# Seven half-size products in place of eight in one block of a split-precision MLP layer

## The chip, the cores and the metric

One NeuronCore of one Trainium2 chip runs the whole program in one launch. The metric is the device time of that launch in microseconds. All arrays come in and go out as fp32.

## What is computed

The reference has three stages. The change lies in the MLP of the second one:

```python
    X = np.fft.fft(x, axis=1)
    X = np.fft.fft(X, axis=2)
    mixed = np.real(X).astype(np.float32)
    u = x + mixed
    mu = np.mean(u, axis=-1, keepdims=True)
    var = np.mean((u - mu) ** 2, axis=-1, keepdims=True)
    un = (u - mu) / np.sqrt(var + 1e-06)
    ch = np.maximum(un @ w_ch1, 0.0) @ w_ch2
    return (u + ch).astype(np.float32)
```

Here x is 2 x 768 x 512 and comes from a block-wise linear attention of 8 heads. w_ch1 is 512 x 2048 and w_ch2 is 2048 x 512. The third stage is a causal convolution gate of 5 taps and two 512 x 512 products.

## The kernel before

Everything is kept transposed: features on the 128 partitions, tokens along the free dimension. The program writes the instruction list of each engine by hand and orders the engines by semaphores.

**Precision.** Each fp32 operand of a large product is split into a rounded high part (an fp32r copy by ScalarE) and a low part (the difference). A product is three matmuls: high x high, low x high, high x low.

**Tiles.** The 1536 tokens form three blocks (`tb`) of 512. The 2048 hidden features form 8 groups (`g`) of 256. A step `m` is one group of one block, so there are 24 steps: 0 to 7 for block 0, 8 to 15 for the middle block, 16 to 23 for block 2.

**TensorE.** `mlp_hidden` (L558) of step m makes 256 hidden features x 512 tokens in banks ps0 and ps1: 2 halves of 12 matmuls with 512 columns. `mlp_out` (L583) of step m makes 4 x 6 matmuls with 512 columns that accumulate in ps4 to ps7 over the 8 groups of a block. In `mlp_step` (L637) the layer 1 of step m+1 is issued ahead of the layer 2 of step m. Banks ps2 and ps3 are free in the MLP but for the Fourier transforms of batch 1 (steps 0 to 3), `mean` and `variance` (L545). The variances of pieces 2 and 3 stand in step 9.

**ScalarE** (`mlp_step`, L858). `hidden_hi` (L799) writes relu(hidden) as fp32r to `hh`. `second_hi` (L767) and `first_hi` (L757) make the high parts of the weights, two and three steps ahead. `cen_hi` (L791) does so for the centred tokens. `squares` (L774), `squares_hi` and `inverse_root` (L784: Ln and Exp, each behind a load of its table) serve the variances.

**VectorE** (`mlp_step`, L1203). `hidden_lo` (L1093) writes the low part of relu(hidden) to `hl`. `centre` (L1060) subtracts the mean. `add_eps` (L1069) reads a variance out of ps2 or ps3, and its semaphore `s_ve` says that the bank is free. `newton` (L1073) refines the inverse root by three instructions on 768 columns. `finish` (L1101) scales the block's result and adds it to `u`.

**GpSimd** makes the low parts of the weights (`first_lo` L1296, `second_lo` L1301), half of those of the centred tokens (`cen_lo` L1306), and `square_sum` and `squares_lo`.

**SyncE** issues the weight loads, each into one of two raw buffers once the splits of that buffer are through.

The lines of layer 1 for one half, with its waits:

```python
                        mm(bank[:, :], w1h[st.slot][:, r, cols], xh, start=r == 0, stop=False)
                        mm(bank[:, :], w1l[st.slot][:, r, cols], xh, start=False, stop=False)
...
                        m = mm(bank[:, :], w1h[st.slot][:, r, cols], cen_l[st.tb][:, r], start=False, stop=r == R - 1)
```

## Time and profile before

| | us |
|---|---|
| median of 3 runs | 429.46 (429.06 to 429.52) |
| the profiled execution, its own time | 428.87 |
| its span, first to last instruction | 426.8 |
| TensorE matmul busy | 421.7 (99% of the span) |
| TensorE weight loads busy | 349.5 (82%) |
| VectorE / ScalarE / GpSimd busy | 244.2 / 173.3 / 189.7 |

An instruction's row in the timeline has its start, its duration, engine, line, operation, operands and count. An ended idle time and its releaser stand in brackets. Matmuls overlap: the distance from one start to the next is what a matmul costs, and its duration is longer. A wait on a semaphore that is already satisfied does not show.

### The profile page before, as it was taken

The page shows a single profiled execution, that of the slowest core. Times are in us where ns is not written, and L with a number is a line of the kernel's source. Part 1 is how long each engine was busy: PE and PEld are TensorE (multiplying, and loading weights), DVE is VectorE, ACT ScalarE, POOL GpSimd, SP SyncE. Part 2 cuts the span into 40 slices and gives each one's busy share as a digit, 9 for nine tenths or more (in the row PEclk, how much of TensorE's full clock was granted, in tenths as well). Part 3 has the DMA queues.
Part 4 walks back from the last instruction along what each step waited for, and adds up shares of the span by engine and source line. Part 5 has one row for each costly group of instructions (what it writes and reads, how often), then busy time and mean ns, then how long its engine had stood idle before and what let it go on. Part 6 is the DMA issues. An engine that isn't in the chain of part 4 may idle for free.

```text
span 426.8 us, 6315 instructions
## 1 busy us (share of the span) xinstructions
PE 421.7 (99%) x2482; PEld 349.5 (82%) x2482; DVE 244.2 (57%) x371; ACT 173.3 (41%) x318; POOL 189.7 (44%) x115
## 2 busy tenths in 40 slices
PE   8999999999999999999999999999999999999997
PEld 7888888788888788888888888888888888888886
DVE  5659999758446341971417101516988859669400
ACT  2355842675203327524262222264254342624212
POOL 3553322344886346986645444445545338300000
PEclk9999999999999999999999999999999999999999
DMA  7987701420331132223232322222321221002022
GB/s 251 356 330 237 224 2 56 141 102 20 129 98 50 51 100 98 98 72 126 93 104 75 117 91 89 89 88 84 105 75 38 99 91 49 0 0 100 0 100 98
DMA packets 14860, 44.06 MB, mean 103 GB/s; under 512 B 1904, under 2 KB 2160, under 8 KB 14832
## 3 DMA queue, kind: packets, MB, share of 16 engines
q1 hardware_dynamic: 14832, 43.67, 30.1%
q8 instruction: 20, 0.33, 0.3%
q14 instruction: 8, 0.07, 0.0%
HBM read 40.52 MB, written 3.15 MB: 102 GB/s over the span
## 4 chain that ended last, share of the span: by engine, by line
PE 96%; DMA 2%; SPq 1%; DVE 1%; ACT 0%; issue 0%
PE ps L572 10%; PE ps L598 10%; PE ps L600 10%; PE ps L599 10%; PE ps L580 10%; PE ps L573 10%; PE ps L487 3%; PE ps L700 3%; PE ps L699 3%; PE ps L698 3%; PE ps L676 3%; PE ps L449 3%; PE ps L677 3%; PE ps L678 3%; PE ps L476 2%; PE ps L531 2%
## 5 line engine op out<-in xcount | busy, mean ns | idle before, releaser
L1097 DVE SCALAR_TENSOR_TENSOR hl<-ps,hh 128x512 fp32r<-128x512 f32 x48 | 32.8, 689 | 114.4 <-ACT hh L805 114.4
L805 ACT ACTIVATE hh<-ps 128x512 fp32r<-128x512 f32 x48 | 28.7, 602 | 160.5 <-PE ps L580 160.5
L1177 DVE SCALAR_TENSOR_TENSOR xT<-u_pad,cw,xT 128x768 f32<-128x768 f32 (+2 forms) x48 | 56.0, 1234 | 0.0
L1304 POOL TENSOR_TENSOR w2l_a<-raw_a,w2h_a 128x1024 fp32r<-128x1024 f32 x12 | 32.2, 2683 | 53.1 <-ACT w2h_a L772 49.6
L1304 POOL TENSOR_TENSOR w2l_b<-raw_b,w2h_b 128x1024 fp32r<-128x1024 f32 x12 | 30.1, 2505 | 55.0 <-ACT w2h_b L772 55.0
L572 PE MATMUL ps<-cen_h,w1h_a 128*128 128x512 f32 x96 | 38.1, 396 | 0.7 <-ACT cen_h L797 0.7
L598 PE MATMUL ps<-hh,w2h_a 128*128 128x512 f32 x96 | 38.2, 398 | 0.0
L598 PE MATMUL ps<-hh,w2h_b 128*128 128x512 f32 x96 | 38.0, 395 | 0.0
L600 PE MATMUL ps<-hh,w2l_b 128*128 128x512 f32 x96 | 37.9, 395 | 0.0
L599 PE MATMUL ps<-hl,w2h_b 128*128 128x512 f32 x96 | 37.9, 395 | 0.0
L573 PE MATMUL ps<-cen_h,w1l_a 128*128 128x512 f32 x96 | 37.7, 392 | 0.0
L572 PE MATMUL ps<-cen_h,w1h_b 128*128 128x512 f32 x96 | 37.6, 392 | 0.0
L573 PE MATMUL ps<-cen_h,w1l_b 128*128 128x512 f32 x96 | 37.5, 391 | 0.0
L600 PE MATMUL ps<-hh,w2l_a 128*128 128x512 f32 x96 | 37.5, 390 | 0.0
L599 PE MATMUL ps<-hl,w2h_a 128*128 128x512 f32 x96 | 37.4, 389 | 0.0
L1299 POOL TENSOR_TENSOR w1l_b<-raw_a,w1h_b 128x1024 fp32r<-128x1024 f32 x12 | 31.0, 2580 | 13.7 <-DVE yy L1034 9.9
L1299 POOL TENSOR_TENSOR w1l_a<-raw_b,w1h_a 128x1024 fp32r<-128x1024 f32 x11 | 30.1, 2734 | 5.1 <-ACT w1h_a L765 5.1
L580 PE MATMUL ps<-cen_l,w1h_a 128*128 128x512 f32 x96 | 26.0, 393 | 0.0
L580 PE MATMUL ps<-cen_l,w1h_b 128*128 128x512 f32 x96 | 25.9, 391 | 0.0
L572 PEld LDWEIGHTS ps<-cen_h,w1h_a 128*128 128x128 f32 x96 | 18.0, 188 | 5.4 <-issue 1.1
L600 PEld LDWEIGHTS ps<-hh,w2l_b 128*128 128x128 f32 x96 | 18.0, 188 | 4.3
L599 PEld LDWEIGHTS ps<-hl,w2h_b 128*128 128x128 f32 x96 | 18.0, 188 | 4.3
(170 smaller groups left out, 936.1 us busy)
## 6 DMA issues: line engine op xcount, KB each, us to landing
raw_a<-in_mlp SPq DMA_DIRECT2D x25, 512.0 KB, 3.6
raw_b<-in_mlp SPq DMA_DIRECT2D x23, 512.0 KB, 3.6
chunks<-in_qkv SPq DMA_DIRECT2D x12, 512.0 KB, 6.6
chunks<-in_qkv SPq DMA_DIRECT2D x22, 256.0 KB, 5.7
out<-out_sb SPq DMA_DIRECT2D x11, 256.0 KB, 2.0
raw_a<-in_val SPq DMA_DIRECT2D x2, 512.0 KB, 3.7
raw_b<-in_out SPq DMA_DIRECT2D x2, 512.0 KB, 4.1
seq_c<-const_seq SPq DMA_DIRECT2D x1, 768.0 KB, 7.7
```

Source lines behind the costliest of these rows:

```text
L449: m = mm(score_bank(n, par)[:, hp * P:(hp + 1) * P], kT[c][rows, hp, :], qT[c][rows, hp, :], start=True, stop=True)
L572: mm(bank[:, :], w1h[st.slot][:, r, cols], xh, start=r == 0, stop=False)
L573: mm(bank[:, :], w1l[st.slot][:, r, cols], xh, start=False, stop=False)
L580: m = mm(bank[:, :], w1h[st.slot][:, r, cols], cen_l[st.tb][:, r], start=False, stop=r == R - 1)
L598: mm(bank[:, :], w2h[st.slot][:, j, r], hh[:, slot, j], start=st.first and j == 0, stop=False)
L599: mm(bank[:, :], w2h[st.slot][:, j, r], hl[:, slot, j], start=False, stop=False)
L600: m = mm(bank[:, :], w2l[st.slot][:, j, r], hh[:, slot, j], start=False, stop=st.last and j == 1)
L805: nc.scalar.activation(hh[:, slot, j], ps[j][:, :], ACT.Relu).then_inc(s_hh, 1)
L1097: stt(hl[:, slot, j], ps[j][:, :], 0.0, hh[:, slot, j].bitcast(F32), ALU.max, ALU.subtract).then_inc(s_hl, 1)
L1177: stt(xT[:, b, r, tok], u_pad[b][:, r, PAD - d + tok.start:PAD - d + tok.stop], cw[:, K - 1 - d, r:r + 1], xT[:, b, r, tok], ALU.mult, ALU ...
L1299: tt(lo, raw_, hi.bitcast(F32), ALU.subtract).then_inc(s_w1l, 1)
L1304: tt(lo, raw_, hi.bitcast(F32), ALU.subtract).then_inc(s_w2l, 1)
```

## The change

In the middle block (steps 8 to 15) layer 1 is computed as a 2 x 2 block product with seven block products. The weights of a group are cut in input halves and in halves of 128 hidden features. The tokens are cut in input halves and in halves of 256 tokens. Four sums of weight blocks (`combine_weights`, per step) and four of token blocks (`combine_tokens`, once) are made in fp32 on VectorE, and then split by ScalarE, VectorE and GpSimd. Each of the seven products is 6 matmuls with 256 columns (42 per step in place of 24 with 512). Four places hold them, each the first 256 columns of ps0 to ps3. `first_products` issues four products, then come two of the four rows of layer 2, then `last_products` with three that accumulate on top of places, then the other two rows. Between them ScalarE keeps the first product (`first_product_kept`), and VectorE adds the shared sums (`first_sums`, `last_sums`). Relu and the low part are then taken over 256 and 768 columns rather than twice 512.

What stands in ps2 and ps3 must be gone by step 8, so the variances of pieces 2 and 3 move from step 9 to step 6, and all that feeds them moves with them. Some other pieces of work move later, and `newton(1)` is spread over three steps. Buffers in SBUF are laid over others (not shown).

```diff
+        def a_block(t, j, d):
+            return t[:, 2 * d:2 * d + 2, j * P:(j + 1) * P]
...
+        def b_block(d, t, lo):
+            return (cen_l if lo else cen_h)[SEVEN][:, 2 * d:2 * d + 2, t * HALF_X:(t + 1) * HALF_X]
...
+        places = [ps[i][:, 0:HALF_X] for i in (*SCORE, COS, SIN)]
...
+            def product(at, a_hi, a_lo, b_hi, b_lo, onto=False):
+                for k in range(2):
+                    mm(at, a_hi[:, k], b_hi[:, k], start=not onto and k == 0, stop=False, skip_group_check=True)
+                    mm(at, a_lo[:, k], b_hi[:, k], start=False, stop=False, skip_group_check=True)
+                    m = mm(at, a_hi[:, k], b_lo[:, k], start=False, stop=k == 1, skip_group_check=True)
+                return m
...
+            def first_products(st):
+                m, w = st.m, nth7(st.m)
+                at1, at6, at7, at5 = places
+                wh_, wl_ = w1h[st.slot], w1l[st.slot]
+                if w == 1:
+                    pe.wait_ge(s_cenl[1], 2 * through[st.tb])
+                    pe.wait_ge(s_cenl[0], through[st.tb] - 1)
+                pe.wait_ge(s_hl, 2 * m if w == 1 else 2 * m - 1)
+                pe.wait_ge(s_w1h, m + 1)
+                pe.wait_ge(s_w1l, m + 1)
+                product(at1, a_block(wh_, 0, 0), a_block(wl_, 0, 0), b_block(0, 0, 0), b_block(0, 0, 1)).then_inc(s_p1, 1)
+                if w == 1:
+                    pe.wait_ge(s_th, 4)
+                    pe.wait_ge(s_tl, 4)
+                pe.wait_ge(s_wsh, 2 * w)
+                pe.wait_ge(s_wsl, 2 * w)
+                for n, at, done, free in ((2, at6, s_p6, s_u2), (3, at7, s_p7, s_c21), (1, at5, s_p5, s_c12)):
+                    if w > 1:
+                        pe.wait_ge(free, w - 1)
+                    elif n == 3:
+                        pe.wait_ge(s_ve, 2 * B)
+                    product(at, s_block(m, n, 0), s_block(m, n, 1), t_block(n, 0), t_block(n, 1)).then_inc(done, 1)
...
+            def last_products(st):
+                m, w = st.m, nth7(st.m)
+                at1, _, at7, at5 = places
+                wh_, wl_ = w1h[st.slot], w1l[st.slot]
+                pe.wait_ge(s_keep, w)
+                product(at1, a_block(wh_, 0, 1), a_block(wl_, 0, 1), b_block(1, 0, 0), b_block(1, 0, 1),
+                        onto=True).then_inc(s_c11, 1)
+                pe.wait_ge(s_v, w)
+                product(at7, a_block(wh_, 1, 1), a_block(wl_, 1, 1), t_block(4, 0), t_block(4, 1),
+                        onto=True).then_inc(s_p74, 1)
+                pe.wait_ge(s_c22, w)
+                product(at5, s_block(m, 4, 0), s_block(m, 4, 1), b_block(1, 1, 0), b_block(1, 1, 1),
+                        onto=True).then_inc(s_h, 2)
...
+                if after and seven(after.m):
+                    first_products(after)
+                    mlp_out(st, (0, 1))
+                    last_products(after)
+                    mlp_out(st, (2, 3))
...
+                if st.m == 6:
+                    variance(2)
+                    variance(3)
...
-                if st.m == 9:
-                    variance(2)
-                    variance(3)
...
+            def combined_hi(m):
+                w = nth7(m)
+                act.wait_ge(s_ws, 4 * w)
+                copy(s_block(m, 1, 0), ws_sum(m, 1)).then_inc(s_wsh, 1)
+                copy(sw_h[m % 2][:, :, :, :], sw_s[m % 2][:, :, :, :]).then_inc(s_wsh, 1)
+            def tokens_hi():
+                act.wait_ge(s_t, 4)
+                copy(t_block(1, 0), t_sum(1)).then_inc(s_th, 1)
+                for n in (2, 3, 4):
+                    copy(t_block(n, 0), t_sum(n)).then_inc(s_th, 1)
+            def first_product_kept(st):
+                act.wait_ge(s_p1, nth7(st.m))
+                if nth7(st.m) > 1:
+                    act.wait_ge(s_u2, nth7(st.m) - 1)
+                copy(p1[:, :], places[0]).then_inc(s_keep, 1)
+            def seven_hi(st):
+                w = nth7(st.m)
+                to = hh[:, st.slot].rearrange("p j n -> p (j n)")
+                act.wait_ge(s_c11, w)
+                act.wait_ge(s_ch, R * (st.m - 1))
+                nc.scalar.activation(to[:, 0:HALF_X], places[0], ACT.Relu).then_inc(s_hh, 1)
+                act.wait_ge(s_c21, w)
+                act.wait_ge(s_c12, w)
+                nc.scalar.activation(to[:, HALF_X:2 * TB], flat_out[:, HALF_X:2 * TB], ACT.Relu).then_inc(s_hh, 1)
             def first_hi(m):
...
+                if after and seven(after.m):
+                    first_product_kept(after)
+                elif after:
                     hidden_hi(after)
...
+                if seven(st.m + 2) and st.m + 2 > FIRST7:
+                    combined_hi(st.m + 2)
...
+                if st.m == 5:
+                    squares_hi(1)
+                if after and seven(after.m):
+                    if st.m == FIRST7 - 1:
+                        inverse_root(1)
+                    if st.m == FIRST7 + 1:
+                        x3_hi(0)
+                    seven_hi(after)
...
+                    squares(2)
+                    squares(3)
+                    tokens_hi()
                 if st.m == 5:
                     inverse_root(0)
+                if st.m == 9:
                     cen_hi(3)
-                if st.m == 6:
-                    squares(2)
-                    squares(3)
-                if st.m == 8:
-                    x3_hi(0)
-                    squares_hi(1)
-                if st.m == 10:
...
+            def combine_tokens():
+                to = [t_sum(n) for n in (1, 2, 3, 4)]
+                (b11, b21), (b12, b22) = ([of_batch(acc_of, i)[:, 2 * d:2 * d + 2] for d in range(2)] for i in (1, 2))
+                dve.wait_ge(s_cen, 6)
+                dve.wait_ge(s_f, 4 * R)
+                tt(to[0], b12, b11, ALU.subtract).then_inc(s_t, 1)
+                tt(to[2], b22, b12, ALU.subtract).then_inc(s_t, 1)
+                dve.wait_ge(s_t, 1)
+                tt(to[1], b22, to[0], ALU.subtract).then_inc(s_t, 1)
+                dve.wait_ge(s_t, 3)
+                tt(to[3], b21, to[1], ALU.subtract).then_inc(s_t, 1)
...
+            def tokens_lo():
+                for n in (1, 2, 3, 4):
+                    dve.wait_ge(s_th, n)
+                    tt(t_block(n, 1), t_sum(n), t_block(n, 0).bitcast(F32),
+                       ALU.subtract).then_inc(s_tl, 1)
...
+            def combine_weights(m):
+                w = nth7(m)
+                raw_ = first_split(m)[0]
+                a11, a12, a21, a22 = (a_block(raw_, j, d) for j in range(2) for d in range(2))
+                to = [ws_sum(m, n) for n in (1, 2, 3, 4)]
+                dve.wait_ge(s_raw1[raw1_slot(m)], raw1_landed(m))
+                dve.wait_ge(s_h, 2 * (m - 1))
+                tt(to[0], a21, a22, ALU.add).then_inc(s_ws, 1)
+                tt(to[2], a11, a21, ALU.subtract).then_inc(s_ws, 1)
+                dve.wait_ge(s_ws, 4 * w - 3)
+                tt(to[1], to[0], a11, ALU.subtract).then_inc(s_ws, 1)
+                dve.wait_ge(s_ws, 4 * w - 1)
+                tt(to[3], a12, to[1], ALU.subtract).then_inc(s_ws, 1)
+            def first_sums(st):
+                w = nth7(st.m)
+                at1, at6, at7, at5 = places
+                if w == 1:
+                    dve.wait_ge(s_mean, 4)
+                else:
+                    dve.wait_ge(s_hh, 2 * st.m)
+                dve.wait_ge(s_keep, w)
+                dve.wait_ge(s_p6, w)
+                tt(u2, at6, p1[:, :], ALU.add).then_inc(s_u2, 1)
+                dve.wait_ge(s_u2, w)
+                dve.wait_ge(s_p7, w)
+                tt(c22, at7, u2, ALU.add).then_inc(s_v, 1)
+                dve.wait_ge(s_v, w)
+                dve.wait_ge(s_p5, w)
+                tt(c22, at5, c22, ALU.add).then_inc(s_c22, 1)
+            def last_sums(st):
+                w = nth7(st.m)
+                at1, _, at7, at5 = places
+                to = hl[:, st.slot].rearrange("p j n -> p (j n)")
+                hi = hh[:, st.slot].rearrange("p j n -> p (j n)")
+                dve.wait_ge(s_hh, 2 * st.m + 1)
+                stt(to[:, 0:HALF_X], at1, 0.0, hi[:, 0:HALF_X].bitcast(F32), ALU.max, ALU.subtract).then_inc(s_hl, 1)
+                dve.wait_ge(s_p74, w)
+                tt(c21, at7, u2, ALU.add).then_inc(s_c21, 1)
+                dve.wait_ge(s_h, 2 * (st.m + 1))
+                tt(c12, at5, u2, ALU.add).then_inc(s_c12, 1)
+                dve.wait_ge(s_hh, 2 * (st.m + 1))
+                stt(to[:, HALF_X:2 * TB], flat_out[:, HALF_X:2 * TB], 0.0, hi[:, HALF_X:2 * TB].bitcast(F32),
+                    ALU.max, ALU.subtract).then_inc(s_hl, 1)
             def hidden_lo(st):
                 slot = st.m % 2
...
+                if after and seven(after.m):
+                    first_sums(after)
+                    if st.m == FIRST7:
+                        add_finished(0)
+                    if st.m in (10, 11, 12):
+                        newton(1, st.m - 10)
+                    if st.m == 13:
+                        cen_lo(3)
+                    last_sums(after)
+                elif after:
                     hidden_lo(after)
+                if st.m == 5:
+                    add_eps(0)
+                    add_eps(1)
+                    tokens_lo()
+                if seven(st.m + 3):
+                    combine_weights(st.m + 3)
                 if st.last:
-                    finish(st.tb)
+                    scale_finished(st.tb)
+                    if st.tb + 1 != SEVEN:
+                        add_finished(st.tb)
                 if st.m == 0:
...
                     centre(3)
-                    cen_lo(2)
-                if st.m == 5:
-                    add_eps(0)
-                    add_eps(1)
+                    combine_tokens()
                 if st.m == 6:
-                    cen_lo(3)
-                    newton(0)
-                if st.m == 9:
-                    x3_lo(0)
                     add_eps(2)
                     add_eps(3)
-                if st.m == 11:
-                    newton(1)
+                    for part in range(3):
+                        newton(0, part)
                 if st.m == 17:
+                    x3_lo(0)
                     x3_lo(1)
...
+                if seven(m):
+                    pool.wait_ge(s_ws, 4 * nth7(m))
+                    tt(lo[:, :, 0:P], raw_[:, :, 0:P], hi[:, :, 0:P].bitcast(F32), ALU.subtract)
+                    tt(a_block(lo, 1, 1), a_block(raw_, 1, 1), a_block(hi, 1, 1).bitcast(F32), ALU.subtract).then_inc(s_w1l, 1)
+                    pool.wait_ge(s_wsh, 2 * nth7(m) - 1)
+                    tt(s_block(m, 1, 1), ws_sum(m, 1), s_block(m, 1, 0).bitcast(F32),
+                       ALU.subtract).then_inc(s_wsl, 1)
+                    pool.wait_ge(s_wsh, 2 * nth7(m))
+                    tt(sw_l[m % 2][:, :, :, :], sw_s[m % 2][:, :, :, :],
+                       sw_h[m % 2][:, :, :, :].bitcast(F32), ALU.subtract).then_inc(s_wsl, 1)
+                else:
...
+                if m == 5:
+                    squares_lo(1)
...
-                if m == 5:
-                    cen_lo(3)
-                if m == 6:
                     square_sum(2)
                     square_sum(3)
-                if m == 8:
-                    squares_lo(1)
+                if m == 9:
+                    cen_lo(3)
```

**ScalarE in step 5 of the program and at the start of step 6.** Before, from `hidden_hi` of step 6 on (`yy`: squares and logarithms; `cen_h`: tokens):

```order
L805 ACTIVATE hh<-ps 128x512 [waits s_ch,s_h]
L805 ACTIVATE hh<-ps 128x512 [waits s_h]
L772 CAST w2h_a<-raw_a 128x1024 [waits s_ch,s_raw2_0]
L765 CAST w1h_a<-raw_b 128x1024 [waits s_h,s_raw1_1]
L787 ACT_TABLE_LOAD
L787 ACTIVATE yy<-yy 128x768 [waits s_ve]
```

And with the change, from `first_hi(8)` on:

```order
L926 CAST w1h_a<-raw_b 128x4x128 [waits s_h,s_raw1_1]
L927 CAST w1h_a<-raw_b 128x2x128
L892 CAST w1h_a<-w1l_a_sums 128x2x128 [waits s_ws]
L893 CAST s_h<-s_l_sums 128x768
L953 ACT_TABLE_LOAD
L953 ACTIVATE yy<-yy 128x768 [waits s_ve]
L955 ACT_TABLE_LOAD
L955 ACTIVATE rstd<-yy 128x768 [waits s_ln]
L974 ACTIVATE hh<-ps 128x512 [waits s_ch,s_h]
L974 ACTIVATE hh<-ps 128x512 [waits s_h]
L938 CAST w2h_b<-raw_b 128x1024 [waits s_ch,s_raw2_1]
```

The two splits of sums, which wait for VectorE's `s_ws`, now stand between the split of the weights and the inverse root, ahead of the relu of step 7 (the first two rows with `hh`).

**VectorE in step 6**, from `hidden_lo` of step 7 on. Before:

```order
L1097 SCALAR_TENSOR_TENSOR hl<-ps,hh 128x512 [waits s_hh] x2
L1086 TENSOR_TENSOR cen_l<-xT,cen_h 128x1024 [waits s_cenh]
L1077 TENSOR_TENSOR yy<-yy,rstd 128x768 [waits s_sd]
L1079 SCALAR_TENSOR_TENSOR yy<-yy,rstd 128x768 [waits s_rstd]
L1081 SCALAR_TENSOR_TENSOR rstd<-yy,rstd 128x768 [waits s_rstd]
```

And with the change:

```order
L1344 SCALAR_TENSOR_TENSOR hl<-ps,hh 128x512 [waits s_hh] x2
L1300 TENSOR_TENSOR w1l_b_sums<-raw_a 128x2x128 [waits s_h,s_raw1_0]
L1301 TENSOR_TENSOR s_l_sums<-raw_a 128x256
L1303 TENSOR_TENSOR s_l_sums<-w1l_b_sums,raw_a 128x256 [waits s_ws]
L1305 TENSOR_TENSOR s_l_sums<-raw_a,s_l_sums 128x256 [waits s_ws]
L1248 TENSOR_SCALAR yy<-ps 128x256 [waits s_var]
L1248 TENSOR_SCALAR yy<-ps 128x512 [waits s_var]
L1255 TENSOR_TENSOR yy<-yy,rstd 128x768 [waits s_sd]
L1258 SCALAR_TENSOR_TENSOR yy<-yy,rstd 128x768 [waits s_rstd]
L1261 SCALAR_TENSOR_TENSOR rstd<-yy,rstd 128x768 [waits s_rstd]
L1317 TENSOR_TENSOR out_sb<-ps,p 128x256 [waits s_p6,s_keep,s_mean]
```

The sums for step 9 and then `add_eps` of pieces 2 and 3, which frees ps2 and ps3, stand behind `hidden_lo` of step 7.

## Rows read from the trace of the kernel before

**Rows 1.** The page: busy time of the engines, and the granted clock in 40 slices.

```profile
PE 421.7 (99%) x2482; PEld 349.5 (82%) x2482; DVE 244.2 (57%) x371; ACT 173.3 (41%) x318; POOL 189.7 (44%) x115
PEclk9999999999999999999999999999999999999999
```

**Rows 2.** The page: the chain that ended last, by engine.

```profile
PE 96%; DMA 2%; SPq 1%; DVE 1%; ACT 0%; issue 0%
```

**Rows 3.** Timeline of TensorE, the variances in step 9 (start us, duration us).

```profile
207.81 0.28 PE L555 MATMUL ps<-square_part,ones_r 128*128 128x256 f32 x1
207.93 0.28 PE L556 MATMUL ps<-square_part,ones_r 128*128 128x256 f32 x1
208.04 0.39 PE L555 MATMUL ps<-square_part,ones_r 128*128 128x512 f32 x1
208.27 0.39 PE L556 MATMUL ps<-square_part,ones_r 128*128 128x512 f32 x1
208.51 0.39 PE L572 MATMUL ps<-cen_h,w1h_b 128*128 128x512 f32 x1
```

**Rows 4.** Timeline of TensorE: first matmuls of layer 1 (L572) and 2 (L598).

```profile
169.24 0.39 PE L598 MATMUL ps<-hh,w2h_a 128*128 128x512 f32 x1
174.69 0.40 PE L572 MATMUL ps<-cen_h,w1h_a 128*128 128x512 f32 x1
...
185.80 0.39 PE L572 MATMUL ps<-cen_h,w1h_b 128*128 128x512 f32 x1
191.26 0.39 PE L598 MATMUL ps<-hh,w2h_a 128*128 128x512 f32 x1
```

**Rows 5.** Timeline of VectorE and of GpSimd in steps 6 and 10.

```profile
175.01 3.04 DVE L1079 SCALAR_TENSOR_TENSOR yy<-yy,rstd 128x768 f32<-128x768 f32 x1
226.38 0.95 DVE L1077 TENSOR_TENSOR yy<-yy,rstd 128x768 f32<-128x768 f32 x1
...
171.05 3.11 POOL L1304 TENSOR_TENSOR w2l_b<-raw_b,w2h_b 128x1024 fp32r<-128x1024 f32 x1 [2.07 <-ACT w2h_b L772]
174.12 3.12 POOL L1299 TENSOR_TENSOR w1l_b<-raw_a,w1h_b 128x1024 fp32r<-128x1024 f32 x1
```

**Rows 6.** Timeline of VectorE, GpSimd and ScalarE in step 4.

```profile
146.66 3.54 DVE L1067 TENSOR_TENSOR xT<-u_pad,ps 128x512 f32<-128x512 f32 x4
150.12 2.23 DVE L1086 TENSOR_TENSOR cen_l<-xT,cen_h 128x512 fp32r<-128x512 f32 x1
...
149.40 2.40 POOL L1299 TENSOR_TENSOR w1l_b<-raw_a,w1h_b 128x1024 fp32r<-128x1024 f32 x1
151.75 1.90 POOL L1310 TENSOR_TENSOR cen_l<-xT,cen_h 128x256 fp32r<-128x256 f32 x2
```

**Rows 7.** Timeline of ScalarE in step 5: the inverse root.

```profile
160.18 1.28 ACT L787 ACT_TABLE_LOAD   x1
161.47 0.85 ACT L787 ACTIVATE yy<-yy 128x768 f32<-128x768 f32 x1
162.34 1.28 ACT L789 ACT_TABLE_LOAD   x1
163.63 0.85 ACT L789 ACTIVATE rstd<-yy 128x768 f32<-128x768 f32 x1
```

**Rows 8.** Groups by line and form: count, busy us, mean ns of one, idle before.

```profile
L580 PEld LDWEIGHTS ps<-cen_l,w1h_a 128*128 128x128 f32 x96 | 18.0, 188 | 4.1
L910 ACT CAST w1h_a<-raw_b 128x512 fp32r<-128x512 f32 x2 | 1.1, 611 | 0.0
L1111 DVE TENSOR_TENSOR xT<-ps,rstd 128x256 f32<-128x256 f32 x8 | 3.0, 420 | 2.0 <-PE ps L600 2.0
L1086 DVE TENSOR_TENSOR cen_l<-xT,cen_h 128x1024 fp32r<-128x1024 f32 x2 | 2.4, 1220 | 0.0
L1117 DVE TENSOR_TENSOR u_pad<-u_pad,xT 128x512 f32<-128x512 f32 x4 | 2.5, 680 | 0.0
L1319 POOL TENSOR_TENSOR yy<-yy 128x512 f32<-128x512 f32 x2 | 2.6, 1289 | 0.2
```

More of the change, by code:

```diff
@@ L91, in sb, with sums_and_low @@
             return sb_in(ctx, name, shape, dt)
+        def sums_and_low(stack, name, shape):
+            with ExitStack() as full:
+                sums = sb_in(full, f"{name}_sums", shape)
+            return sums, sb_in(stack, name, shape, F32R)
         ps = [ctx.enter_context(nc.psum_tensor(f"ps{i}", [P, 512], F32)) for i in range(8)]
@@ L112, in program @@
         cen_h0, cen_h1 = (sb(f"cen_h{i}", [P, R, TB], F32R) for i in range(2))
-        cen_l0, cen_l1 = (sb(f"cen_l{i}", [P, R, TB], F32R) for i in range(2))
+        cen_s1, cen_l1 = sums_and_low(ctx, "cen_l1", [P, R, TB])
+        with ExitStack() as first_low:
+            cen_l0 = sb_in(first_low, "cen_l0", [P, R, TB], F32R)
+        with ExitStack() as combined_weights:
+            s_h1 = sb_in(combined_weights, "s_h1", [P, 3, 2, P], F32R)
+            s_s1, s_l1 = sums_and_low(combined_weights, "s_l1", [P, 3, 2, P])
+        sb("first_low_rest", [P, R * TB])
         with ExitStack() as att:
@@ L162, in program @@
         sb("region3_rest", [P, NC * YW])
+        u2 = flat_out[:, 0:HALF_X]
+        c12, c21, c22 = (flat_out[:, i * HALF_X:(i + 1) * HALF_X] for i in (1, 2, 3))
+        sw_h, sw_l, sw_s = [s_h0, s_h1], [s_l0, s_l1], [s_s0, s_s1]
         raw = [raw_a, raw_b]
@@ L584, in mlp_out @@
+            def mlp_out(st, rows=range(R)):
                 pe.wait_ge(s_hh, 2 * (st.m + 1))
@@ L591, in mlp_out @@
                 pe.wait_ge(s_w2l, st.m + 1)
-                for r in range(R):
+                for r in rows:
                     if st.first and st.tb:
@@ L796, in cen_hi @@
                     act.wait_ge(s_cen, 2 * i + e + 1)
+                    if i == 2 and e == 0:
+                        continue
                     copy(of_block(cen_h, i)[:, pair], of_batch(acc_of, i)[:, pair]).then_inc(s_cenh, 1)
@@ L1112, in finish, with add_finished @@
                            ALU.mult).then_inc(s_fin, 1)
+            def add_finished(tb):
                 for i in pieces_of[tb]:
```

90 lines of the change are left out of this document (65 added, 25 removed).

## The prediction

> **What bounds the kernel now.** The page comes first. TensorE is busy for 99% of the span at the full granted clock of 2.4 GHz in every slice, while VectorE and GpSimd are near a half [rows 1]. The chain that ended last runs through TensorE for 96% [rows 2]. So in the MLP every matmul taken away is worth its full distance to the next, as long as TensorE never waits; and every wait that the change adds is paid in full. The forecast is a difference of these two sums. An effect of under 0.2% (0.86 us) cannot be told from no change here.
>
> **The gain.** In the variances two matmuls with 256 columns take from 207.81 to 208.04, 0.23 us, and one with 512 takes 0.23 too (208.04 to 208.27) [rows 3]. Each of them has its own weight load, so half a product costs half. Layer 1 of a step, 24 matmuls, takes 5.46 us (185.80 to 191.26) [rows 4]. The change issues 42 halves, or 21 of 24: 7/8 of 5.46 is 4.78, a gain of 0.68 us per step and 5.5 us in 8 steps. Layer 2 is unchanged: 24 matmuls in 5.45 us (169.24 to 174.69) [rows 4].
>
> A rule speaks of this term: the Trainium skill, TensorE: Matmul & The Clock Gate, "Back-to-back issue gap", gives N/2.4 + 2.5 ns. By it 42 x 109.2 ns against 24 x 215.8 ns would gain 0.59 us per step, 4.7 us in all. The 512-column distance measured here, 230 ns, is longer than its 216.
>
> **What one thing costs beside another.** VectorE and GpSimd do not work side by side when VectorE reads both inputs from SBUF. Such an instruction on 768 columns took 0.95 us at 226.38, and 3.04 us at 175.01, when GpSimd ran from 174.12 to 177.24 [rows 5]: it waited 2.2 us for the end of GpSimd's instruction, and GpSimd's (3.12 us, where 2.40 is usual) had waited for the one before it. So they alternate, one whole instruction each. Prices without the wait: VectorE 0.42 us for 256 columns, 0.68 for 512, 1.22 for 1024; ScalarE 0.61 for 512 [rows 8] and 0.85 for 768 [rows 7]; GpSimd 1.29 for 512 [rows 8], 2.40 for 1024 [rows 6]. From these I estimate by straight line 0.4 us for ScalarE's 256 columns and 0.7 and 1.85 us for GpSimd's 256 and 768. Instructions that do not wait for each other start some 0.1 us closer than they last: four of 3.54 us together in [rows 6].
>
> **The entry, steps 4 to 8.** All times are on the trace's clock.
> - Step 4. `centre` ends at 150.1 as before [rows 6]. `combine_tokens`, four times 512 columns from SBUF, replaces one such instruction. GpSimd holds on until 151.8, then has two of 256, and `square_sum`, which now follows here. Alternating, the four end at about 156.5. GpSimd's `square_sum` of both pieces ends at 160.9.
> - ScalarE waits with `tokens_hi` for all four sums, and its relu of step 6 stands behind it. Four copies of 0.5 us end at 158.8, relu at 159.8, the split for layer 2 at 160.7. TensorE doesn't need this relu before layer 1 of step 7, at 163.8 (169.24 less 5.46 [rows 4]), so nothing is lost yet. Then come `squares_hi(1)` and `first_hi(8)`, to 162.4.
> - VectorE does `hidden_lo`, `add_eps` and `tokens_lo` (four times 512; the first two wait for GpSimd's low weights and `squares_lo(1)`) to 167.2, then `combine_weights(8)`, four times 256: 168.8.
> - ScalarE splits these sums (0.3 + 0.8) to 169.9 and makes `inverse_root(0)`: 4.3 us with its two table loads [rows 7], to 174.1. Before, it ran at 160.18. The relu of step 7 follows at 175.2, `hidden_lo` at 176.1.
> - TensorE would start the products of step 8 at 175.4: layer 2 of step 6 now starts after variances of 0.7 us, 169.94 + 5.45 [rows 3, 4]. They wait for `hidden_lo`: **0.7 us lost**.
> - VectorE then makes `combine_weights(9)`. Its first instruction is free, the second waits for GpSimd's low weights of layer 2 (2.40). It ends at 179.9, and only then `add_eps` of pieces 2 and 3 frees ps2 and ps3, at 180.9. TensorE has done two products (1.4 us) by 177.5, and the third writes ps2: **3.5 us lost**. This is the largest new wait.
> - Behind it VectorE has `newton(0)`, three times 768 columns in turns with GpSimd, to 184.9, and then two sums before `s_v`, at 185.9. TensorE comes there at 185.9: 0.1 us lost.
> - In step 8 VectorE has `add_finished(0)` between the sums. Its two instructions of 1.13 us wait for two of GpSimd, to 200.3. `hidden_lo` of the first 256 columns is behind it, at 200.7, where TensorE is ready at 200.4: 0.4 us with the restart.
>
> **The steady steps.** After the last product of a step the sum, relu over 768 columns and low part over 768 take 0.4 + 0.8 + 0.9 us and the crossings, at most 2.4 more behind GpSimd: 5 us. Layer 2 asks for it 2 rows (2.73 us) and four products (2.74 us) later, at 5.5. So this is covered by layer 2; without that cover the 5 us would be bare. GpSimd has 1.25 + 0.65 + 0.65 + 1.8 + 2.36 = 6.7 us per step, VectorE's SBUF pairs 1.4 + 0.85, and up to 0.9 for a part of `newton(1)`: 9 to 9.9 us in turns, and a step lasts 4.78 + 5.45 = 10.2. I take 0.5 us for step 11, where `cen_lo(3)` (2.5 us) puts the low weights of layer 2 behind. The SP queue's weight loads wait for the same splits as before; each buffer has a step to spare. `x3_lo(0)`, moved to step 17, is 2.3 us on VectorE (two times 1.22 less the overlap [rows 8]). In block 2 a low part is asked for by 5.5 us of layer 2 after its relu, which hides it; without that cover it would be 2.3 us bare. I cost it at nothing, and so the other moved pieces, which stand under the same layers.
>
> **The sum.** Gain 5.5; waits 0.7 + 3.5 + 0.1 + 0.4 + 0.5 = 5.2. Against the profiled execution, 428.87 (2.07 us of it outside its span of 426.8), this makes 428.6; the median shown is 0.6 us above that execution, so 429.2 us against 429.46. The bounds of the waits: 0 if the turns did not add up along the entry, and 5.2 + 2.4 if one more instruction of the chain lands behind one of GpSimd's of 2.40 us. I stay with 5.2, since [rows 5] show the turns as a rule. This case by itself holds 427.6 to 430.8.
>
> **The rivals.**
> - *The entry is shorter.* If the sums fall where GpSimd is idle, the bank is free by about 178 and the waits shrink to some 1.5 us: 425.5 us. For it: GpSimd is busy for only 44% overall [rows 1]. Against it: in step 4 its work from 149.40 on leaves no gap [rows 6], and `square_sum` now follows it. 17%.
> - *Turns bound every step (the other side).* VectorE and GpSimd together have 9 to 9.9 us of exclusive work in a step of 10.2. It decides once this passes 10.2: each of GpSimd's four pieces with 0.15 us more of start and crossing gives 10.7 in the steps with extras, and the wait moves into `s_v`, the low weights or `hl`. 0.5 us in each of 8 steps adds 4: 433 us. For it: GpSimd's splits of 1024 columns already stretch from 2.40 to 3.1 us beside VectorE [rows 5, 6]. Against it: in the steps without extras 9.0 leaves over 1 us. 13%.
> - *The clock falls.* TensorE stood still nowhere before, and the clock stayed at 2.4 GHz [rows 1]; a wait of 3.5 us has no precedent in this trace. At 1.2 GHz the next 2.7 us of products take twice as long: 432 us. 6%.
> - *Half products cost more than half.* A weight load lasts 188 ns [rows 8], more than the 115 of a half matmul. If it set the pace, 42 x 0.188 = 7.9 us instead of 5.46 would add 2.4 us per step: 19 more, 449 us. The pair in [rows 3] speaks against it, though it is only two matmuls, and on one and the same weight block. The Trainium skill, Perfetto Trace Analysis, "Matmuls", says that larger matmuls are more efficient than smaller ones. 3%.
> - *The change doesn't do what it says*: if the eighth were not saved, only the waits would stand, 434 us. The order shows 42 half matmuls per step in place of 24 whole ones, so 1%.
>
> **How the numbers follow.** The forecast has 60%. Of it, 0.20 falls below 428.6, 0.27 within 0.2% and 0.13 above 430.3. With the first rival (0.17) on the fast side and the other four (0.23) on the slow one: faster 0.37, same 0.27, slower 0.36. Both signs are near even, since gain and waits are two numbers of one size. The range of 8 in 10 goes from 426.0 to 432.5: it takes in half of the first rival and most of the clock case.
>
> **What would show it.** Right: 336 matmuls with 256 columns at 0.115 us in the middle block, layers of 4.8 us; one idle of TensorE near 178 of about 3.5 us, released by VectorE's `add_eps`; one of 0.7 us before it; instructions of VectorE with SBUF pairs at 2 to 3 us beside GpSimd. The clock full throughout. Wrong: no idle at `s_ve`, idle in each of steps 9 to 15, or a distance above 0.12 us between half matmuls.

## The result and the profile after

| | before | after |
|---|---|---|
| median, us (lowest to highest, runs) | 429.38 (429.06 to 430.79, 12) | 430.76 (429.95 to 432.42, 12) |
| the profiled execution, its own time | 428.87 | 430.34 |
| its span | 426.8 | 428.6 |

The changed kernel takes 1.0038 of the time before, 95% interval 1.0023 to 1.0054: slower by 0.38%. The forecast was 429.2, no change that can be told, from a gain of 5.5 us and waits of 5.2 us. The time lies within the range given (426.0 to 432.5), on the slow side.

The page of the changed kernel, its engines and its chain, against [rows 1, 2]:

```profile
PE 418.7 (98%) x2626; PEld 353.0 (82%) x2626; DVE 283.6 (66%) x450; ACT 185.9 (43%) x353; POOL 210.2 (49%) x139
PEclk9999999999999999999999999999999999999999
PE 75%; DVE 14%; ACT 3%; POOL 3%; issue 2%; DMA 2%; SPq 1%; ACTq 0%; DVEq 0%; POOLq 0%
```

TensorE's count rises by 144: 8 steps of 42 half matmuls in place of 24 whole ones. Its busy time falls by only 3.0 us, and a fifth of the chain no longer runs through it. From 146 to 181 us, up to the wait for the bank, the chain runs almost wholly through VectorE and ScalarE. From 188 to 225 us, up to the wait in step 11, GpSimd comes in too, and from 293 to 309 us, in block 2, it is VectorE.

TensorE's waits in the stretches that the change touches (engine, tile, line, releaser: us in total, times, longest); the four left out lie before step 7:

```profile
PE ps L665 <- DVE yy L1248: 2.8, 1, 2.8
...
PE ps L665 <- issue: 0.5, 1, 0.5
...
PE ps L652 <- DVE hl L1344: 0.3, 1, 0.3
PE ps L723 <- POOL w2l_b L1578: 0.3, 1, 0.3
```

The entry of block 1 in the timelines of TensorE, VectorE, ScalarE and GpSimd, to set against [rows 4, 5, 7]:

```profile
176.57 0.36 PE L665 MATMUL ps<-cen_h,w1h_a 128*128 128x256 f32 x1 [0.48 <-issue]
181.00 0.39 PE L665 MATMUL ps<-t_h,s_h 128*128 128x256 f32 x1 [2.77 <-DVE yy L1248]
...
175.07 1.29 DVE L1344 SCALAR_TENSOR_TENSOR hl<-ps,hh 128x512 fp32r<-128x512 f32 x2 [6.01 <-ACT hh L974]
176.28 0.42 DVE L1300 TENSOR_TENSOR w1l_b_sums<-raw_a 128x256 f32<-128x256 f32 x1
176.61 2.61 DVE L1301 TENSOR_TENSOR s_l_sums<-raw_a 128x256 f32<-128x256 f32 x1
179.93 1.02 DVE L1248 TENSOR_SCALAR yy<-ps 128x256 f32<-128x256 f32 x2
...
170.26 1.28 ACT L953 ACT_TABLE_LOAD   x1
174.46 1.06 ACT L974 ACTIVATE hh<-ps 128x512 fp32r<-128x512 f32 x2
...
176.54 2.40 POOL L1578 TENSOR_TENSOR w2l_b<-raw_b,w2h_b 128x1024 fp32r<-128x1024 f32 x1 [2.83 <-ACT w2h_b L938]
```

Read from the bottom up, it is the chain of the prediction. The square roots hold ScalarE from 170.26, so the relu of step 7 comes at 174.46 and its low part at 175.07. VectorE's second sum of weights (L1301, 256 columns) starts just behind GpSimd's 2.40 us and takes 2.61. `add_eps` (L1248) frees the bank at 180.9, and TensorE stands for 2.77 us.

The price of a half product is in these rows of TensorE, from the first matmul of a piece of layer 1 to the first of layer 2 behind it:

```profile
190.27 0.28 PE L665 MATMUL ps<-cen_h,w1h_b 128*128 128x256 f32 x1
193.14 0.40 PE L723 MATMUL ps<-hh,w2h_a 128*128 128x512 f32 x1
195.89 0.28 PE L665 MATMUL ps<-cen_h,w1h_b 128*128 128x256 f32 x1
198.04 0.40 PE L723 MATMUL ps<-hh,w2h_a 128*128 128x512 f32 x1
```

24 halves take 2.87 us and 18 take 2.15: 5.02 us for the 42. In every other step it is 2.82 and 2.14 us (243.69 to 246.51, 249.30 to 251.44), 4.96. On average a half takes **0.119 us**, where the prediction had 0.114 and 4.78 us a step. Layer 1 of before takes 5.46 and 5.52 us in turn (the 5.52 is 174.69 to 180.21 of its timeline). The gain is best read over two whole steps without a wait, layer 2 included. From layer 1 of step 13 to that of step 15 it is 21.07 us (233.17 to 254.24), before 22.02 (230.53 to 252.55). That is 0.47 us per step, 3.8 in eight, not 5.5.

Where the rest of the 1.8 us of span comes from is told by two rows of each kernel, layer 1 of step 7 and of step 16 (L572 before, L652 after):

```profile
163.78 0.40 PE L572 MATMUL ps<-cen_h,w1h_b 128*128 128x512 f32 x1
263.46 0.40 PE L572 MATMUL ps<-cen_h,w1h_a 128*128 128x512 f32 x1
```

```profile
164.30 0.40 PE L652 MATMUL ps<-cen_h,w1h_b 128*128 128x512 f32 x1
264.76 0.40 PE L652 MATMUL ps<-cen_h,w1h_a 128*128 128x512 f32 x1
...
309.60 0.47 PE L652 MATMUL ps<-cen_h,w1h_a 128*128 128x512 f32 x1 [0.26 <-DVE hl L1344]
```

| stretch | after less before, us |
|---|---|
| up to step 7 (inputs landed later in this execution; the change is not there yet) | +0.52 |
| steps 7 to 15 | +0.78 |
| step 16 to the end (the wait at 309.60, and a slower restart) | +0.50 |

In steps 7 to 15 a gain of 3.8 meets losses of 4.5: 0.6 before 176.57, 3.1 around the bank, 0.3 in steps 8 and 9, 0.5 in step 11.

The span grows by 1.8 us in these two executions, the time by 1.5. What an execution takes outside its span is 2.0 to 2.2 us in every one of the kernel before and of its variants, and 1.7 to 1.8 in every one of the changed kernel and of its variants: some 0.35 us less. No run shows why.

### The profile page after: what moved, and what is told of

Same layout as the page of the kernel before. It is cut to its first block, busy times and chain, and to the rows that moved or that the text cites. A ratio compares the mean times of both kernels' runs of the same rounds, so it can differ in the third digit from the quotient of the medians.

```text
span 428.6 us, 6824 instructions
## 1 busy us (share of the span) xinstructions
PE 418.7 (98%) x2626; PEld 353.0 (82%) x2626; DVE 283.6 (66%) x450; ACT 185.9 (43%) x353; POOL 210.2 (49%) x139
## 4 chain that ended last, share of the span: by engine, by line
PE 75%; DVE 14%; ACT 3%; POOL 3%; issue 2%; DMA 2%; SPq 1%; ACTq 0%; DVEq 0%; POOLq 0%
PE ps L723 7%; PE ps L725 7%; PE ps L724 7%; PE ps L652 6%; PE ps L660 6%; PE ps L653 6%; PE ps L567 3%; PE ps L831 3%; PE ps L830 3%; PE ps L829 3%; PE ps L807 3%; PE ps L529 3%; PE ps L808 3%; PE ps L809 3%; PE ps L556 2%
## 5 line engine op out<-in xcount | busy, mean ns | idle before, releaser
L1344 DVE SCALAR_TENSOR_TENSOR hl<-ps,hh 128x512 fp32r<-128x512 f32 x32 | 21.6, 688 | 57.6 <-ACT hh L974 57.6
L974 ACT ACTIVATE hh<-ps 128x512 fp32r<-128x512 f32 x32 | 18.9, 601 | 93.3 <-PE ps L660 93.3
L1573 POOL TENSOR_TENSOR w1l_b<-raw_a,w1h_b 128x1024 fp32r<-128x1024 f32 x8 | 20.6, 2580 | 18.1 <-DVE yy L1211 9.9
L652 PE MATMUL ps<-cen_h,w1h_a 128*128 128x512 f32 x64 | 25.6, 399 | 1.0 <-ACT cen_h L966 0.7
L652 PE MATMUL ps<-cen_h,w1h_b 128*128 128x512 f32 x64 | 25.2, 393 | 0.0
L653 PE MATMUL ps<-cen_h,w1l_a 128*128 128x512 f32 x64 | 25.1, 393 | 0.0
L653 PE MATMUL ps<-cen_h,w1l_b 128*128 128x512 f32 x64 | 25.0, 391 | 0.0
L1573 POOL TENSOR_TENSOR w1l_a<-raw_b,w1h_a 128x1024 fp32r<-128x1024 f32 x7 | 19.4, 2768 | 5.1 <-ACT w1h_a L931 5.1
L723 PEld LDWEIGHTS ps<-hh,w2h_b 128*128 128x128 f32 x96 | 18.0, 188 | 4.3 <-issue 0.4
L725 PEld LDWEIGHTS ps<-hh,w2l_a 128*128 128x128 f32 x96 | 18.0, 188 | 3.9
```

Source lines behind the costliest of these rows:

```text
L723: mm(bank[:, :], w2h[st.slot][:, j, r], hh[:, slot, j], start=st.first and j == 0, stop=False)
L725: m = mm(bank[:, :], w2l[st.slot][:, j, r], hh[:, slot, j], start=False, stop=st.last and j == 1)
L974: nc.scalar.activation(hh[:, slot, j], ps[j][:, :], ACT.Relu).then_inc(s_hh, 1)
L1344: stt(hl[:, slot, j], ps[j][:, :], 0.0, hh[:, slot, j].bitcast(F32), ALU.max, ALU.subtract).then_inc(s_hl, 1)
L1573: tt(lo, raw_, hi.bitcast(F32), ALU.subtract).then_inc(s_w1l, 1)
```

## The experiments

All were timed beside the kernel before on the same chip.

**The changed kernel again (e0).** No edit.

> The changed kernel once more, as a common measure for the runs beside it. Both theories on its time expect 430.2 to 430.6 us in executions with the full granted clock. Theory 'the wait for the bank lets the clock fall': some executions show a mean granted clock of 0.996 and 1.5 to 2 us more, as 5 of 12 did (431.9 to 432.4 us). Theory 'these are stray executions': none of that kind, or as many in the kernel before.

431.94 us (431.67 to 432.75, 5 runs) against 429.82: ratio 1.0055 (1.0041 to 1.0069). That is 1.2 us above the first measurement. All five executions had a mean granted clock of 0.996. So had five of the twelve first ones, and those took 431.93 to 432.42 us, the other seven 429.95 to 431.04. None of the 16 executions of the kernel before beside it was below 0.999. The profile shows where the clock fell; the view gives, for each stretch, its length, the busy time and count of each engine, the clock, and DMA share and rate:

```profile
181.03 0.39 PE L665 MATMUL ps<-t_h,s_h 128*128 128x256 f32 x1 [2.76 <-DVE yy L1248]
182.79 0.63 PE L723 MATMUL ps<-hh,w2h_b 128*128 128x512 f32 x1
183.22 0.63 PE L724 MATMUL ps<-hl,w2h_b 128*128 128x512 f32 x1
...
181.00:182.00 1.00, 0.97 (x8) 0.98 (x9) 1.00 (x1) 1.00 (x2) 1.00 (x2) 1.00 0.82 250
183.00:184.00 1.00, 1.00 (x3) 0.79 (x3) 0.96 (x2) 0.99 (x2) 1.00 (x1) 0.50 0.08 12
186.00:190.00 4.00, 4.00 (x28) 3.64 (x27) 1.52 (x4) 1.14 (x3) 3.15 (x2) 1.00 0.03 10
```

The wait of 2.76 us ends at 181.03. TensorE works at the full clock for another 1.2 us, and from about 182.2 to 185.6 the granted clock is 0.50, that is 1.2 GHz. Matmuls of 512 columns came 0.43 us apart instead of 0.23. From the end of the wait to the next piece of layer 1 it is 5.85 us (181.03 to 186.88), where the profiled execution of the changed kernel at the full clock has 4.29 (181.00 to 185.29): 1.6 us more.

**Eight products in halves (e1).** The kernel before, with block 1's layer 1 as 48 halves:

```
-    xh = cen_h[st.tb][:, r]
-    mm(bank[:, :], w1h[st.slot][:, r, cols], xh, ...)
+    for t in [slice(0, TB // 2), slice(TB // 2, TB)]:      # in block 1
+        xh = cen_h[st.tb][:, r, t]
+        mm(bank[:, t], w1h[st.slot][:, r, cols], xh, ...)
```

> The kernel before with layer 1 of the middle block as 48 matmuls of 256 columns per step in place of 24 of 512, and nothing else; it computes the same. Theory A, a half matmul in a long row of them costs 0.1195 us wherever it stands: layer 1 takes 48 x 0.1195 = 5.74 us against 5.48, 0.25 us more per step, 2.0 us in all, 431.3 us. Theory B, it costs 0.115, and the longer distance of the changed kernel comes from what else the change adds (sums on VectorE, waits, places): 5.5 us, no difference, 429.4 us.

431.17 us (430.77 to 431.68, 6 runs): ratio 1.0032 (1.002 to 1.0043), +1.35 us. This kernel saves no product and adds no wait; the halves alone cost this. Steps 7 to 15 take 101.51 us in its trace, before 99.68. Theory A holds.

```profile
186.93 0.28 PE L574 MATMUL ps<-cen_h,w1h_b 128*128 128x256 f32 x1
192.68 0.40 PE L600 MATMUL ps<-hh,w2h_a 128*128 128x512 f32 x1
198.15 0.28 PE L574 MATMUL ps<-cen_h,w1h_a 128*128 128x256 f32 x1
203.81 0.39 PE L600 MATMUL ps<-hh,w2h_b 128*128 128x512 f32 x1
```

48 take 5.75 and 5.66 us, 0.119 each, against 5.46 and 5.52 for 24 whole ones. The pair of halves in [rows 3] was no measure: 0.23 us for two, from starts rounded to 0.01 us, allows anything from 0.110 to 0.120.

**The bank freed first (e2).** In step 6 VectorE does `add_eps(2)` and `add_eps(3)` ahead of `hidden_lo(7)`.

> The changed kernel with add_eps of pieces 2 and 3 ahead of hidden_lo of step 7 on VectorE; their variances are done 4 us before. The wait of 3.0 us for the bank must go. Theory 'the bank is what is late': 3.0 us less, 427.3 us. Theory 'VectorE as a whole is late': the sums of step 8 stand behind newton(0), which ends only 0.9 us sooner at most, so TensorE waits for s_v some 2.3 us later on instead, and 0.6 to 0.9 us are gained: 429.6 us. With the wait cut to under 2.5 us the executions with a clock of 0.996 should go, if the wait makes them.

430.76 us (430.12 to 431.11, 11 runs): ratio 1.0021 (1.0013 to 1.003). The wait did not go, it moved:

```profile
PE ps L665 <- DVE out_sb L1320: 2.0, 1, 2.0
...
PE ps L665 <- DVE hl L1331: 0.6, 1, 0.6
```

L1320 is the sum before `s_v`. So the place of `add_eps` is not the cause; VectorE as a whole is late. The executions at 0.996 did not go, against the expectation: five of the eleven had that clock, with no wait above 2.0 us in the profile. They took no longer than the others (430.45 to 431.11). None of them has a trace, and why it cost nothing there is open.

**The square roots a step later (e3).** One character:

```
-                if st.m == 5:
+                if st.m == 6:
                     inverse_root(0)
```

> The changed kernel with inverse_root(0) on ScalarE one step later, behind the relu and the splits of step 7, in front of the kept product. The relu of step 7 then follows the split of the sums at 170.3 rather than at 174.5 on the trace's clock, and everything on VectorE behind it comes 4 us sooner. My theory of the entry (one chain ScalarE to VectorE to bank): the waits of 0.5 and 3.0 us both go and none replaces them, 3.5 us less, 426.8 us in all executions, with the full clock. Rival (GpSimd and VectorE in turns are full here anyway): the waits shrink by half at most and reappear at s_v or at the low parts of the weights, 428.5 us.

428.08 us (427.08 to 428.57, 5 runs): ratio 0.9958 (0.9945 to 0.9971), every clock 0.999 or more. It is faster than both kernels, 3.9 us below e0 in the same comparison, where all of e0's executions had the slow stretch of the clock. In the profiles steps 7 to 15 take 97.78 us (165.10 to 262.88), 2.7 less than in the changed kernel. My theory had both waits gone and 426.8 us; one of 0.8 us stayed. A second time, on another chip, beside f2:

> The kernel of e3 a second time, on this chip beside f2: 1.5 to 2.1 us below the kernel before if e3's gain is its own and not its chip's; no execution at a mean clock of 0.996, because its longest TensorE wait is 0.8 us.

427.77 us (427.5 to 428.53, 5 runs) against 429.75: ratio 0.9956 (0.9943 to 0.9968). Its waits in the stretch:

```profile
PE ps L665 <- DVE yy L1248: 0.8, 1, 0.8
PE ps L652 <- DVE hl L1344: 0.3, 1, 0.3
PE ps L723 <- POOL w2l_b L1578: 0.2, 1, 0.2
```

So VectorE was late because it waited for ScalarE's relu of step 7, 6.01 us in the rows above, and that stood behind 4.3 us of square roots.

**The wait filled (f0).** The changed kernel, with 20 half matmuls whose result nobody reads between the second product of step 8 and the wait for the bank:

```
+    if w == 1 and n == 2:
+        for k in range(20):
+            last = mm(ps[1][:, HALF_X:TB], s_block(m, 2, 0)[:, k % 2],
+                      t_block(2, 0)[:, k % 2], start=True, stop=True, ...)
```

> The changed kernel with 20 more matmuls of 128 by 256 into the unused half of bank 1, between the second product of the first seven-product step and the wait for bank 2 (their result is read by nobody; they cost nothing while they fit in the 2.8 us wait: 20 x 0.12 = 2.4 us). Theory A, the clock falls because TensorE stood still for 2.8 us: no execution has a mean clock of 0.996, all lie where the changed kernel's undisturbed ones lay, about 430.3 us (429.9 to 431.0), and the half-clock stretch of 3.4 us is gone from the profile. Theory B, the fall has another cause: executions at 0.996 and 431.9 us go on at about the same share (5 of 12, and 5 of 5, so far). The filler also tells whether the wait is what the timeline says: if it were shorter than 2.4 us in most executions, the time would rise by the difference.

430.41 us (430.08 to 430.88, 11 runs): ratio 1.0016 (1.0007 to 1.0025), every clock 0.999 or 1.0. What is left of the wait:

```profile
178.27 2.56 PE L695 MATMUL ps<-t_h,s_h 128*128 128x256 f32 x20
181.23 0.39 PE L665 MATMUL ps<-t_h,s_h 128*128 128x256 f32 x1 [0.40 <-DVE yy L1253]
```

TensorE does 2.4 us more work and ends no later. The time is that of the seven executions of the changed kernel at the full clock. This speaks for the standing still as what lets the clock fall. It doesn't settle it: f0 ran on another chip than e0, the unfilled changed kernel was not run beside it, and a chip on which the clock doesn't fall isn't ruled out. The fall costs about 1.7 us: 432.07, the median of the ten executions of the changed kernel at 0.996, less 430.34, that of its seven at the full clock.

**Quarters (f1).** As e1, with four parts of 128 columns.

> The kernel before, with layer 1 of block 1 as 96 matmuls of 128 columns per step in place of 24 of 512 (same products, same weights, banks and waits). Theory A, a constant per matmul: 512 columns at 0.2287 us and 256 at 0.1191 make 0.0095 us + 0.428 ns a column, so 128 columns take 0.0643 us, 96 of them 6.17 us a step against 5.49, eight steps +5.5 us: about 435.3 us. Theory B, below some width the weight load sets the pace: the distance stays near the half matmul's 0.119, 96 of them 11.4 us a step, +47 us: about 477 us. Anything between them prices the weight load, which the half-width products were just wide enough to hide.

471.42 us (470.93 to 471.89, 4 runs): ratio 1.0968 (1.0953 to 1.0983), +41.7 us. Far from theory A's 5.5, and nearly theory B's 47.

```profile
191.83 0.22 PE L574 MATMUL ps<-cen_h,w1h_b 128*128 128x128 f32 x1
202.50 0.45 PE L600 MATMUL ps<-hh,w2h_a 128*128 128x512 f32 x1
```

96 take 10.67 us: 0.111 each, hardly less than a matmul of twice the width. Something other than the columns sets this pace.

**Narrow weights (g1, g2).** e1 and f1 with weights of 64 columns: `cols = slice(j * P, j * P + P // 2)` and `bank[0:64, t]`. Both leave out half of block 1's hidden values.

> The kernel with eight products in halves (e1), but every weight of layer 1 of block 1 with 64 columns in place of 128: it leaves out half of the hidden values of that block, so its time is that of the same 48 matmuls of 256 columns a step behind narrower weight loads. Theory A, the surplus of the half matmul (0.119 us, where half of a full one is 0.114) is the weight load's: the distance falls to 0.107 to 0.114, which takes 384 x 0.005 to 0.012 = 1.9 to 4.6 us off e1's 431.2: 426.6 to 429.3 us. Theory B, it is a constant of every matmul: the distance stays at 0.119 and the time at 431.2 us.

> The kernel with quarters (f1, 0.111 us a matmul of 128 columns), with weights of 64 columns as in g1, so it too leaves out half of the hidden values of block 1. Theory A, the 0.111 is the load of 128 weight columns: 64 of them load in about half of it, and the stream with its constant takes over at 0.064 us: about 435 us. Theory B, it is a fixed price of a load or of a matmul, whatever its width: 0.111 and 471 us as in f1.

```profile
187.22 0.28 PE L577 MATMUL ps<-cen_h,w1h_b 128*64 128x256 f32 x1
192.67 0.39 PE L603 MATMUL ps<-hh,w2h_a 128*128 128x512 f32 x1
198.14 0.28 PE L577 MATMUL ps<-cen_h,w1h_a 128*64 128x256 f32 x1
203.74 0.39 PE L603 MATMUL ps<-hh,w2h_b 128*128 128x512 f32 x1
```

```profile
187.46 0.22 PE L577 MATMUL ps<-cen_h,w1h_b 128*64 128x128 f32 x1
193.22 0.44 PE L603 MATMUL ps<-hh,w2h_a 128*128 128x512 f32 x1
```

Halves: 429.65 us (429.28 to 430.74, 11 runs), ratio 1.0002 (0.9994 to 1.0011); 48 take 5.45 and 5.60 us, 0.115 each. Quarters: 432.68 us (432.28 to 433.07, 5 runs), ratio 1.007 (1.0057 to 1.0082); 96 take 5.76 us, 0.060 each. Theory A holds for the quarters, which halve their distance. For the halves the direction is its own, but 0.115 us and 429.65 lie just above what it gave (0.107 to 0.114, at most 429.3). So the 0.111 is the load of 128 weight columns, and with a load half as wide a half matmul comes down to about half of a whole one. Whether the whole one would come down too was still open. The Trainium skill (TensorE: Matmul & The Clock Gate, "LDWEIGHTS (loading the stationary operand)") has a load take its columns over 1.2, in ns, that is 107 for 128 columns and 53 for 64. The runs agree, with 111 for 128; for 64 they give only an upper bound of 60.

**Narrow weights, whole matmuls (h1).** As g1, with matmuls of 512 columns; it too leaves out half of block 1's hidden values.

> The kernel before, with 64 weight columns in place of 128 for layer 1 of block 1 and its matmuls whole (512 columns); it leaves out half of the hidden values of that block. It is the missing reference of g1: there a half matmul with narrow weights took 0.115 us, against 0.119 with wide ones. Theory A, every matmul has a constant on top of its columns, and it is smaller behind a narrow load (0.005 against 0.009 us): 24 whole ones take 5.39 us a step in place of 5.49, 8 steps make -0.8 us: about 428.9 us. Theory B, the surplus is there only where columns and load are about equal (256 columns), and a whole matmul doesn't feel its load: 5.49 us a step and 429.7 us as the kernel before.

```profile
174.91 0.39 PE L577 MATMUL ps<-cen_h,w1h_a 128*64 128x512 f32 x1
180.44 0.39 PE L603 MATMUL ps<-hh,w2h_b 128*128 128x512 f32 x1
```

429.78 us (429.44 to 430.3, 11 runs) against 429.73: ratio 1.0006 (0.9997 to 1.0015). 24 take 5.53 us, 0.230 each, no less than with wide weights. Theory B holds: a whole matmul doesn't feel its load, and with narrow weights a half costs half, 0.115 of 0.230. The surplus of the half with wide weights is the load's alone.

**Uneven parts (g3).** As e1, with 320 and 192 columns.

> The kernel with layer 1 of block 1 in matmuls of 320 and 192 columns in place of 256 and 256. Theory A, linear in the width down to where it costs what a weight load costs (0.111 us, from f1): 320 columns 0.1465, 192 columns 0.111 in place of 0.092, a pair 0.2575 against 0.238, 192 pairs +3.7 us over e1: about 434.9 us. Theory B, linear down to 192 columns and the load's floor only below: as e1, 431.2 us.

435.44 us (434.81 to 435.78, 4 runs): ratio 1.013 (1.0115 to 1.0146), near theory A's 434.9. The first half of a step, 12 matmuls of 320 columns and then 12 of 192:

```profile
211.47 0.31 PE L574 MATMUL ps<-cen_h,w1h_b 128*128 128x320 f32 x1
213.23 0.25 PE L574 MATMUL ps<-cen_h,w1h_b 128*128 128x192 f32 x1
214.55 0.33 PE L574 MATMUL ps<-cen_h,w1h_b 128*128 128x320 f32 x1
```

The twelve of 320 take 1.76 us, 0.147 each, and the twelve of 192 take 1.32, 0.110 each. The 192 columns cost what 128 do. 256 columns lie just beside this: 0.115 us of their own (g1), and 0.111 for the load. My reading is that neither hides the other fully there, hence 0.119; no run shows the overlap itself.

**The entry spread out (f2).** e3, and: `add_eps(2)` and `add_eps(3)` before `combine_weights(9)`; `add_finished(0)` in two pieces, steps 8 and 9, with `x3_hi(0)` one step later; `x3_lo(0)` in step 16.

```
+                if st.m == 6:
+                    add_eps(2)
+                    add_eps(3)
                 if seven(st.m + 3):
                     combine_weights(st.m + 3)
...
-                    if st.m == FIRST7:
-                        add_finished(0)
+                    if st.m in (FIRST7, FIRST7 + 1):
+                        add_finished(0, (st.m - FIRST7,))
...
                 if st.m == 6:
-                    add_eps(2)
-                    add_eps(3)
...
+                if st.m == 16:
+                    x3_lo(0)
                 if st.m == 17:
-                    x3_lo(0)
                     x3_lo(1)
```

> The changed kernel with the square roots of batch 0 one step later (as in e3), and besides: the two banks freed before the sums of the weights, the 5.5 us of adding the finished block 0 split over steps 8 and 9 (its fp32r copy on ScalarE moved from step 9 to 10), and the low part of the finished block 0 taken in step 16 in place of 17. Theory A, what is left of waits in e3 (0.8 us for the bank, 0.4 for the low part of step 8's hidden values, 0.4 in block 2) goes and nothing else comes: 1.2 to 1.6 us below e3, about 426.7 us. Theory B, VectorE as a whole is the limit through step 7 and the early freeing of the banks only moves the wait to s_v, as it did in e2: 0.4 to 0.8 us below e3, about 427.4 us.

**425.95 us** (425.72 to 426.23, 4 runs) against 429.75: ratio 0.9911 (0.9897 to 0.9924), 3.8 us below the kernel before and the best of all. It is 1.8 us below e3 in the same comparison, somewhat more than theory A gave; the profile's list of waits has none of TensorE from step 7 on.

```profile
164.34 0.40 PE L652 MATMUL ps<-cen_h,w1h_b 128*128 128x512 f32 x1
260.65 0.40 PE L652 MATMUL ps<-cen_h,w1h_a 128*128 128x512 f32 x1
```

Steps 7 to 15 take 96.31 us, before 99.68: 3.4 us less. 0.4 us is still lost between the products of step 8: the matmul at 182.59 starts 0.42 us after the one before it, just behind VectorE's sum before `s_v` (L1320, 182.11 to 182.53). Together they are the gain of the seven products by itself, 8 x 0.47 = 3.8. That the median too fell by 3.8 is chance: it is the 3.4, and 0.35 outside the span.

## Why the prediction was wrong, by its own steps

- **The gain: this step failed.** "Each of them has its own weight load, so half a product costs half", from the pair in [rows 3]. A half matmul costs 0.119 us, not 0.114, and 42 of them 5.0 us, not 4.78. The term measured 3.8 us (0.47 per step in the steps without a wait), not 5.5. The fourth rival had the mechanism, the weight load, but priced it by its duration of 188 ns [rows 8]; loads overlap one another, and their pace is 0.111 us (f1). (Its 449 us also leaves out the waits of 5.2.) The signs for telling it were too lax as well: "a distance above 0.12" would have let 0.119 pass as 0.115. The rule of the Trainium skill (TensorE: Matmul & The Clock Gate, "Back-to-back issue gap") leaned the right way with 4.7 us. But the Trainium skill gives it for an isolated matmul, without a weight load; its 109 ns is 119 in the trace.
- **The turns of VectorE and GpSimd: right.** A sum of 256 columns took 2.61 us behind one of GpSimd's of 2.40, as [rows 5] had shown.
- **The entry: right in place, a little long.** Predicted 0.7, 3.5, 0.1 and 0.4 us; found 0.6, 3.1, 0.0 and 0.3. The chain by hand (relu of step 7 at 174.1, bank free at 180.9) met 174.46 and 180.9, though the whole trace lay 0.5 us later, so the work in it was that much shorter. Step 11: predicted 0.5, found 0.5. Together 4.5 against 5.2.
- **The moved pieces at nothing: wrong for one.** `x3_lo(0)` in step 17 stands ahead of taps and of the low part that TensorE waits for at 309.60: 0.5 us. I had named its cover, 5.5 us of layer 2, but had put against it one piece of 2.3 us alone. VectorE's queue held low parts (the first row here, before the second) and then 5.9 us of taps. The third low part made them 4.4 us longer, not 2.3. In f2, with this piece in step 16, step 16 to the end is as long as before (163.35 us, before 163.34).

```profile
293.98 9.01 DVE L1434 TENSOR_TENSOR cen_l<-u_pad,cen_h 128x2048 fp32r<-128x2048 f32 x3
...
292.68 4.57 DVE L1183 TENSOR_TENSOR cen_l<-u_pad,cen_h 128x1024 fp32r<-128x1024 f32 x2
```

- **The third rival, the clock, came true in ten of seventeen executions** of the changed kernel (5 of 12 and 5 of 5), at a price of 1.7 us. That 432.07 meets the rival's own 432 is luck: its price of 2.7 was too high, and the time that it was added to, 429.2, too low. Its premise was too strong as well: the trace of before has waits of TensorE too, the longest 1.1 us. It had 6%, as a case that would either come or not. It comes in some executions and not in others, and so belonged into the sum with a share.
- **The second rival, turns in every step: did not come.** TensorE loses 0.3 us in steps 8 and 9 and 0.5 in step 11, and nothing from 12 to 15.
- **Outside the span: carried over.** The prediction took the 2.07 us of before; it is 1.7, some 0.35 less.

The sum as it should have stood: -3.8 + 4.5 + 0.5 - 0.35 = +0.85 us at the full clock. The seven first executions at the full clock have a median of 430.34, 1.0 us above before; with the five others it is 1.4.

## What to carry to other kernels

In these runs, with one load per matmul, a matmul costs the longer of its stream and its weight load, and a little more than either where the two are about equal. Before splitting products into halves, see what width the load allows. With 128 weight columns a matmul of 256 costs 4% more than half of one of 512. One of 192 or 128 costs nearly as much as one of 256, so below 256 hardly anything is saved (no width between 192 and 256 was run). When a change moves work between engines, the first step of the new regime deserves the most care: here eight steps gained 3.8 us and the entry took it all back, and moving one call (`inverse_root(0)`) by a step returned 2.7 of it. And a wait of TensorE of some 3 us needs a second price with a share, for the clock behind it: here 1.7 us in ten of seventeen executions.
